# A ring of eight raw weight chunks, all splits in an expert's first slot, and experts taken alternately large and small

## What is computed

```python
# attention with 8 heads over chunks of 32 tokens, then a mixing layer -> x (2, 768, 512)
logits = x @ w_gate                                  # (2, 768, 8)
local_gate = sigmoid(x @ w_local)
for b in range(2):
    prev_e = -1
    for s in range(768):
        fresh_e = argmax(logits[b, s])
        e = fresh_e if s == 0 or local_gate[b, s] < 0.5 else prev_e
        prev_e = e
        p = softmax(logits[b, s])
        out[b, s] = p[e] * (relu(x[b, s] @ w1[e]) @ w2[e])
```

## Time and profile before

| | us |
|---|---|
| median of 3 runs | 558.23 |
| the runs | 552.83, 558.23, 558.38 |
| span of the profiled execution | 553.9 |
| TensorE matmul busy | 446.1 (81%) |
| VectorE busy | 247.3 (45%) |
| ScalarE busy | 214.1 (39%) |
| GpSimd busy | 50.8 (9%) |
| mean granted TensorE clock | 0.910 |

### The profile page before, as it was taken

The page is one execution under the profiler, slowest core; times in us unless marked ns, Lnnn a source line. Parts: engine busy times, 40 slices in busy tenths (PEclk is TensorE's granted clock), DMA queues, the critical chain, the costliest instruction groups (busy, mean ns, idle before and its releaser), DMA issues.

```text
span 553.9 us, 10631 instructions
## 1 busy us (share of the span) xinstructions
PE 446.1 (81%) x3759; PEld 368.3 (66%) x3760; DVE 247.3 (45%) x478; ACT 214.1 (39%) x320; POOL 50.8 (9%) x62
## 2 busy tenths in 40 slices
PE   1757639999999999999500589999899989898772
PEld 1645529798989989898300467777678767676552
DVE  2545576544425344431451455222642364646661
ACT  1333466635243343431111453223432345435640
POOL 0000000010101010100035001111111101111010
PEclk9887759999999999999755679999999999999987
DMA  8687533272000000000057845111551155554640
GB/s 316 220 284 245 199 122 112 72 279 103 0 0 0 0 0 0 0 1 2 0 159 229 292 161 197 63 47 30 185 194 38 38 190 179 188 178 148 217 161 10
DMA packets 18309, 67.26 MB, mean 121 GB/s; under 512 B 2734, under 2 KB 2734, under 8 KB 18288
## 3 DMA queue, kind: packets, MB, share of 16 engines
q1 hardware_dynamic: 13104, 50.92, 27.2%
q0 software_dynamic: 4896, 16.05, 8.5%
q10 hardware_dynamic: 288, 0.02, 0.0%
HBM read 55.41 MB, written 12.62 MB: 123 GB/s over the span
## 4 chain that ended last, share of the span: by engine, by line
PE 54%; DMA 17%; issue 9%; DVE 8%; ACT 4%; POOL 2%; DVEq 2%; ACTq 2%; SPq 1%; POOLq 0%
PE PS L407 12%; PE PS L534 10%; PE PS L439 10%; PE PS L517 7%; DMA QK<-tiles 5%; PE PS L423 5%; DMA XR<-grouped_rows 4%; DMA ERAW<-wexp 3%; DVE ELO L1036 2%; POOL grouped_rows L1131 2%; DMA rows_out<-OSB,OIDX 2%; PE PS L525 2%; PE PS L457 2%; ACT EHI L701 2%; PE PS L334 1%
## 5 line engine op out<-in xcount | busy, mean ns | idle before, releaser
L1036 DVE TENSOR_TENSOR ELO<-ERAW,EHI 128x1024 f32 (+1 forms) x56 | 66.6, 1222 | 40.3 <-ACT EHI L701 23.0
L701 ACT ACTIVATE EHI<-ERAW 128x1024 f32 (+1 forms) x56 | 56.8, 1052 | 42.6 <-DMA ERAW<-wexp 31.4
L517 PE MATMUL PS<-EHI,XSH 128*128 128x512 f32 x128 | 55.1, 430 | 7.7 <-DVE XSL L1044 7.7
L534 PE MATMUL PS<-EHI,HH 128*128 128x512 f32 x128 | 54.8, 428 | 5.6 <-DVE ELO L1036 4.9
L407 PE MATMUL PS<-XHI,WHI 128*128 128x256 f32 x192 | 56.5, 294 | 1.2 <-DVE WLO L819 1.2
L1057 DVE TENSOR_TENSOR HL<-PS,HH 128x512 fp32r<-128x512 f32 x32 | 22.1, 690 | 76.3 <-ACT HH L721 76.3
L407 PE MATMUL PS<-XLO,WHI 128*128 128x256 f32 x192 | 55.1, 287 | 0.0
L407 PE MATMUL PS<-XHI,WLO 128*128 128x256 f32 x192 | 55.1, 287 | 0.0
L517 PE MATMUL PS<-ELO,XSH 128*128 128x512 f32 x128 | 52.6, 411 | 0.0
L517 PE MATMUL PS<-EHI,XSL 128*128 128x512 f32 x128 | 52.6, 411 | 0.0
L534 PE MATMUL PS<-ELO,HH 128*128 128x512 f32 x128 | 50.6, 395 | 0.0
(11 more groups left out here) (144 smaller groups left out, 760.4 us busy)
## 6 DMA issues: line engine op xcount, KB each, us to landing
ERAW<-wexp SPq DMA_DIRECT2D x56, 512.0 KB, 4.4
QK<-tiles SPq DMA_DIRECT2D x12, 768.0 KB, 5.7
VV<-tiles SPq DMA_DIRECT2D x12, 520.0 KB, 3.7
grouped_rows<-ZR POOLq DMA_DIRECT2D x1, 5140.0 KB, 18.3
RAW<-wmix SPq DMA_DIRECT2D x10, 512.0 KB, 3.8
XR<-grouped_rows POOLq DMA_DIRECT2D x17, 257.0 KB, 3.1
CO<-consts SPq DMA_DIRECT2D x1, 470.0 KB, 5.3
rows_out<-OSB,OIDX POOLq DMA_INDIRECT x16, 2.8
```

Of the source, the lines that this page charges most:

```text
L517: last = nc.tensor.matmul(PS[part][:, :], x[:, k, :], ww[:, c:c + 512], start=n == 0, stop=n == 11)
L534: last = nc.tensor.matmul(PS[4][:, :], x[:, f, :], ww[:, c:c + D], start=n == 0, stop=n == 23)
L701: nc.scalar.activation(EHI[w][:, ds(j * CH2, CH2)], ERAW[i][:], ACT.Copy).then_inc(ehi_done, 1)
L1036: nc.vector.tensor_tensor(ELO[w][:, ds(j * CH2, CH2)], ERAW[i][:], EHI[w][:, ds(j * CH2, CH2)].bitcast(F32), ALU.subtract).then_inc(elo_do ...
```

## The change

Three things, in one diff.

1. The ring has eight buffers, one for each chunk (NRAW = 8). To make room, the slots' working tiles (`XSH`, `XSL`, `HS`, `HH`, `HL`, `OSB`) lie over `X2R`, whose rows have been scattered when they are first written. The first expert's eight loads are all issued at once; none waits for `xr_loaded`. ScalarE and VectorE split all eight, then do `x_hi(0)` and `x_lo(0)`. From then on a buffer is loaded again when its chunk of the expert before has been split.
2. All eight splits of the next expert stand in slot k = 0, whatever n is, in six places on ScalarE and five on VectorE, each within `If(k < ahead)`. `ahead` is a new table entry (`following`), 1 if the next position has an expert with tiles. It is read from `RT` along with `slots_of`'s two; the sum `total` and the nested `If`s go.
3. The position of an expert is no longer its rank r but min(2r, 2U - 1 - 2r), U being the number of experts with tiles: largest, smallest, second largest, second smallest and so on. With these inputs: 5, 1, 4, 1, 2, 1, 2 tiles. This takes seven more linked instructions, and the new table entry one more and a copy.

Beside these, the wait for `meta_done` moves from the end of `x_lo` to the start of `meta_now`.

```diff
-NRAW = 4
+NRAW = 8
@@ SyncE
-            def expert_load(e, which, c, first):
+            def expert_load(e, which, c, first, first_expert=False):
...
-                else:
+                elif not first_expert:
                     sp.wait_ge(elo_done, N2 * e + c + 1 - NRAW)
...
             for c in range(N2):
-                if c == NRAW:
-                    sp.wait_ge(xr_loaded, 16)
-                expert_load(0, x, c, c < NRAW)
+                expert_load(0, x, c, c == 0, True)
@@ all engines
+        def following(eng, e):
+            return eng.value_load(RT[0:1, ds(e + 3 * NE + 1, 1)], min_val=0, max_val=1)
@@ ScalarE
             for c in range(N2):
-                if c == NRAW:
-                    x_hi(0)
-                expert_hi(0, c, c // NRAW, c % NRAW, 0)
+                expert_hi(0, c, 0)
+            x_hi(0)
...
+                def next_hi(k, *chunks):
+                    if split:
+                        with act.If(k < ahead):
+                            if chunks[0] == 0:
+                                act.wait_ge(y_done, first + 1)
+                            for c in chunks:
+                                expert_hi(e + 1, c, 1 - w)
...
+                        next_hi(k, 0, 1)
                         relu_part(s, 0)
+                        next_hi(k, 2)
                         h_hi(s, 0)
+                        next_hi(k, 3)
                         relu_part(s, 1)
+                        next_hi(k, 4)
                         h_hi(s, 1)
+                        next_hi(k, 5)
                         x_hi(s + 1)
+                        next_hi(k, 6, 7)
@@ VectorE, routing
-            link(tt(placed, outer(rank), sq(CO[:, C_POS:C_POS + NE * NE]), ALU.is_equal))
+            used, both, spot = RN[0][:, NE:NE + 1], RN[1][:, 0:NE], RN[9][:, 0:NE]
+            link(ts(both, nt, 0.0, None, ALU.is_gt))
+            link(red(used, both, AX.X, ALU.add))
+            link(ts(both, rank, used, -2.0, ALU.subtract, ALU.mult))
+            link(ts(both, both, -1.0, None, ALU.add))
+            link(nc.vector.scalar_tensor_tensor(both, rank, 2.0, both, ALU.mult, ALU.min))
+            link(nc.vector.scalar_tensor_tensor(spot, rank, used, rank, ALU.is_ge, ALU.mult))
+            link(tt(spot, spot, both, ALU.max))
+            link(tt(placed, outer(spot), sq(CO[:, C_POS:C_POS + NE * NE]), ALU.is_equal))
...
+            link(ts(RN[8][0:1, 0:NE - 1], RN[6][0:1, 1:NE], 0.0, None, ALU.is_gt))
+            nc.vector.tensor_copy(RT[0:1, 3 * NE + 1:4 * NE], RN[8][0:1, 0:NE - 1])
@@ VectorE, first expert and slots
             for c in range(N2):
-                if c == NRAW:
-                    x_lo(0)
-                expert_lo(0, c, c % NRAW, 0)
+                expert_lo(0, c, 0)
+            x_lo(0)
...
+                        next_lo(k, 0, 1)
                         h_lo(s, 0)
+                        next_lo(k, 2, 3)
                         h_lo(s, 1)
+                        next_lo(k, 4)
                         x_lo(s + 1)
+                        next_lo(k, 5)
                         dve.wait_ge(y_done, s + 2)
                         dve.wait_ge(osb_free, s + 1)
                         nc.vector.tensor_scalar(OSB[:], PS[4][:, :], META[:, 0:1], None,
                                                 ALU.mult).then_inc(out_ready, 1)
                         nc.vector.tensor_copy(OIDX[:], META[:, 1:2]).then_inc(oidx_done, 1)
+                        next_lo(k, 6, 7)
                         dve.wait_ge(oidx_done, s + 1)
                         meta_now(s + 1)
```

## The result

The changed kernel takes **560.28 us** (median of 20 runs, 557.5 to 563.2), the kernel before in the same comparison 556.46 (20 runs, 552.7 to 560.0). The ratio is **1.0072, 95% interval 1.0051 to 1.0093**: slower by 0.7%, or 3.8 us. The spans of the profiled executions are 560.6 and 553.9 us, 6.7 us apart.

What follows compares the result with a forecast made beforehand. It took the start, slot 0 and the stalls of slots 1 to 15 to decide: 10.6 − 7.0 − 3.9 = −0.3 us, applied to the median 558.23, predicting 558 us, range 549 to 568.

Steps and rivals of the forecast that it cites:

- Routing, +1.8: Before the table and scatter: eight more linked instructions and a copy delay the start by 1.8 us.
- Start, +10.6: Up to slot 0's first matmul: scatter and XR share DMA with the weights, 10.6 us later, routing included.
- turns: At the start: scatter and weights queues alternate once both have work, so the scatter gets half; sum +10.6 us.
- the two bounds: Start's limits: scatter at its old pace and only XR pays, +4.4 us; or weights go first, +20.5 us.
- Rivals 1 and 2: At the start: scatter not held up, 551.7 us, chance 0.22; or weights go first, 567.8 us, chance 0.20.
- Slot 0, −7.0: First slot: all chunks split before XR, leaving one low-clock start; 15.3 us long, 7.0 us less.
- (a): Slots 5, 10, 13, first slots after one without splits: TensorE waits 2.1 us each, 6.3 in all.
- (b): Slots 6, 11, directly behind a one-tile expert's first slot: TensorE waits 4.6 us each, 9.2 in all.
- slot 14: Slot behind the last split slot: no splits, same VectorE chain, h_lo late by 2.0 us.
- (c): Slots without splits behind split slots: 2.0 us of wait in slot 14, 0 in slots 1, 7 and 12.
- Rival 3: TensorE's clock falls in the 4.6 us waits, 1.5 us lost twice: +3.0 us, 560.9; chance 0.16.
- Rival 4: Slots 1 to 15: the reordering brings nothing, stalls stay 21.4 us, total 562; chance 0.10.

Runs made afterwards that it cites:

- early_xr: Changed kernel with each XR load issued ahead of the output scatter it stood behind; 553.13 us, ratio to the kernel before 0.9940.
- half_w: Changed kernel loading only the first half of each weight chunk from the second expert on; 552.38 us, ratio to the kernel before 0.9922.
- before_early: Kernel before, with each XR load issued ahead of the previous slot's output scatter; 555.98 us, ratio to the kernel before 0.9984.
- order_undone: Changed kernel with experts in sorted order, routing instructions kept; 562.46 us, ratio to the kernel before 1.0117.
- order_alone: Kernel before with only the new expert order and its routing, ring of four and old split places kept; 567.79 us, ratio to before 1.0199.
- two: Changed kernel with the second expert's loads held until the first XR landed and XR loads ahead of output scatters; 547.08 us, ratio to before 0.9837.
- meta_first: Changed kernel with META's update placed ahead of splits 6 and 7 on VectorE; 566.97 us, ratio to the kernel before 1.0162.
- three: Changed kernel with the edits of two and meta_first together; 540.26 us, ratio to the kernel before 0.9698.
- three_sorted: The kernel three with experts in sorted order, routing instructions kept; 543.45 us, ratio to the kernel before 0.9753.

## Why the prediction was wrong, step by step

It forecast no change (−0.3 us); the kernel got 3.8 us slower. Its likeliest case was wrong in sign, within what it called 1% and within its range. That 558 lies only 2.3 us from 560.28 is luck in part. It stands on a median of three runs, 558.23, where 20 runs give 556.46, and it took the profiled execution for one of the lowest by comparing its span, 553.9, with device times; the span of an execution is 1.7 us shorter, so it was an ordinary one.

- **Routing, +1.8**: right. From the last X2T to the start of the table's last copy are 15.83 us (268.82 to 284.65) against 14.02 before.
- **Start, +10.6**: right, 11.1. The choice of turns over the two bounds held: 51.9% and 51.1% of the engines in 300 to 304, XR landing at about 318.6, where its transposes begin. Rivals 1 and 2 are out. The Trainium skill (DMA: Bandwidth & Descriptors, Queues, rings and completion order) says that each engine goes round its queues; the trace agrees for a stretch in which both queues have long had packets. In the first few us it doesn't agree: there the later queue moved next to nothing (286 to 288 before, 339.6 to 342 after). The prediction saw that silence, counted it once at the start, and didn't ask where else a scatter is issued into a running weights' queue. It also counted a chunk as 128 packets, where the queue's count, small packets included, is 576 for four (282 to 303 in the kernel before), 144 each; that makes its upper bound 3.6 us too low and changes nothing in the forecast.
- **Slot 0, −7.0**: right. From its first matmul to slot 1's (336.46) are 15.31 us, forecast 15.3, and no wait for HS.
- **(a), (b) and slot 14, 17.5 us of waits**: the places right, each oversized: 1.0 for 2.1, 4.1 and 3.65 for 4.6, 1.04 for 2.0; 11.8 in all, 5.7 less than forecast. This hid half of what the next two terms cost. From META's copy in slot 6 (407.06) to the next split are 3.91 us, 3.76 before; but I had added a table read and taken the delay from where VectorE had been, not from what TensorE still had to do.
- **(c) "Slots 1, 7, 12 ... 0"**: this is the step that failed, 6.5 us of waits for XR put at nothing. I followed VectorE's chain there (META, table read, `h_lo`) and found it on time. It was. What came late was XR, behind an output scatter behind weights. In the kernel before, chunks were reloaded as four and four over two slots, and XR was late by 0.8 us at most; with all eight in one slot, they pile up just when GpSimd sends the output. That this made the 6.5 us is shown by early_xr, half_w and before_early. I had asked what the freed buffers trigger only at the start; the question stood in each of the six split slots.
- **Rival 3, the clock, 0.16, +3.0 us**: the mechanism was there, 4.7 us: in slots 6 and 11 behind waits of 4.1 and 3.65 as it said (1.5 each, its own figure), and in slot 12 behind the XR wait. With (c) it is the other term that the sum put at nothing. It should have been part of the forecast: the only wait that the prediction had for the clock to hold was one of 1.84 us, and it forecast waits of 4.6. The Trainium skill (TensorE: Matmul & The Clock Gate, Part 1) says that an idle stretch returns the clock to half rate. In the changed kernel the trace agrees for the waits of 4.08 and 3.65 us and for that of 2.19 in slot 12, and not for those of 2.09 and 2.21 in slots 1 and 7, behind which the clock stayed full.
- **Rival 4, "the reordering brings nothing: stalls stay 21.4"**: this came nearest by its number (23.3), for other reasons. In slots 1 to 15 the order gave nothing against the sorted one (order_undone), but it isn't the cause either.
- **The end, 0**: it was −1.2. From the last output scatter's issue to the end are 8.05 us before and 6.8 after. Behind the last OSB the kernel before has 9.7 us, before_early 9.4, all the others 8.4 to 8.7, order_alone among them, which has the old splits. Why is open.

In sum 11.1 − 6.9 + 2.2 − 1.2 + 1.5 = 6.7, the 1.5 being the untouched part. The stalls of slots 1 to 15 were forecast at 17.5 and are 11.8 + 6.5 + 4.7, with 0.3 in small pieces 23.3. Had (c) held, slots 1 to 15 would have taken 215.4 − 6.5 − 1.8 (slot 12's clock) = 207.1; early_xr measured 206.5, and was faster than before.

## What to carry to other kernels

When a change bunches transfers, list every other transfer that is issued while they run, and what is queued behind it on its engine; here the loss sat in a load that no edit touched, behind a store that no edit touched. Issue what the bottleneck waits for ahead of what nobody waits for (XR ahead of the output), and do it before shortening anything else: the same edit (META's update) cost 5 us without it and gave 7 with it, since one wait had covered another. And a wait of about 4 us of TensorE (3.65 to 4.08 here) is to be priced at its length and 1.2 to 2.7 us more, by slots 6 and 11 of the changed kernel and of two.

## What the runs showed of the hardware that I had not expected

- A scatter by GpSimd that was issued while weight chunks were queued moved one packet in the 2.4 us behind its generation (339.6 to 342), where one without weights beside it began within 0.9 us (355.0 to 355.5 behind 354.56). From 342 to 343 it had 58% of the engines, the weights 42%. With the chunks at half their size, the load behind it came 1.8 us earlier.
- GpSimd's generation of one output scatter takes 1.01 to 1.03 us with none of VectorE's splits beside it. Beside two splits it takes 1.21 to 1.23 in the changed kernel and 1.77 to 1.81 in meta_first and three, where META's update stands ahead of the splits. What makes the difference isn't shown.
- The clock fell behind waits of 1.8 us in three_sorted and held behind the same in three. In the changed kernel it held behind waits of 2.09 and 2.21 us and fell behind one of 2.19. The length of the wait alone doesn't decide it.
